# A two-layer feed-forward part behind local attention: the up projection by seven products of half blocks

## The reference

```python
# attention, B=4, H=8, S=576, D=64: pooled attention over groups of 4 positions,
# repeated 4 times, plus attention over the band |i-j| < 4
x = attn_out.transpose(0, 2, 1, 3).reshape(2304, 512)
h = x @ w_in                    # 512 -> 2048
g = np.where(h > 0.0, h, np.exp(np.minimum(h, 0.0)) - 1.0)
x = g @ w_out                   # 2048 -> 512
h = x @ w_in2                   # 512 -> 2048
r = np.maximum(h, 0.0)
out = (s * (r * r) + b) @ w_out2
```

## Time and profile before

| | us |
|---|---|
| median of 3 runs (lowest, highest) | 928.75 (927.66, 928.97) |
| the profiled execution | 932.17 |
| its span | 930.4 |
| PE busy in the span | 905.8 |
| DVE, ACT, POOL busy | 396.3, 413.1, 148.3 |

### The profile page before, as it was taken

One profiled execution on the slowest core, in us unless ns is written; L12 is line 12 of the kernel. 1 busy time (PEld: TensorE's weight loads), 2 busy tenths in 40 slices (PEclk: granted clock), 3 DMA queues, 4 the chain that ended last, 5 costly groups with the idle time before them and its releaser, 6 DMA issues.

```text
span 930.4 us, 16164 instructions
## 1 busy us (share of the span) xinstructions
PE 905.8 (97%) x5936; PEld 853.6 (92%) x5936; DVE 396.3 (43%) x774; ACT 413.1 (44%) x1104; POOL 148.3 (16%) x148
## 2 busy tenths in 40 slices
PE   5898999999999999999999999999999999999998
PEld 5777789999999999999999989899998999999896
DVE  6788844233233233232333453443443443443433
ACT  8889976544344343344466432232232332322222
POOL 5565647300000000000156400000000000000000
PEclk9889999999999999999999999999999999999999
DMA  8987534200000000000044200000000000000000
GB/s 196 206 199 195 131 100 135 62 1 1 1 0 0 0 0 0 0 1 1 23 125 125 69 1 0 35 1 1 35 0 0 34 0 0 35 1 1 34 1 35
DMA packets 42929, 41.47 MB, mean 45 GB/s; under 512 B 3616, under 2 KB 30080, under 8 KB 42880
## 3 DMA queue, kind: packets, MB, share of 16 engines
q1 hardware_dynamic: 42880, 40.83, 16.7%
HBM read 36.09 MB, written 4.72 MB: 44 GB/s over the span
## 4 chain that ended last, share of the span: by engine, by line
PE 90%; SPq 2%; issue 2%; POOL 2%; DVE 2%; ACT 1%; DMA 1%; POOLq 0%; ACTq 0%; DVEq 0%
PE ps_h L517 43%; PE ps_y L538 22%; PE ps_y L536 21%; PE ps_t L450 1%; PE ps_sd L435 1%; POOL v L371 1%; SPq L243 1%; PE ps_xd L479 1%; PE ps_s L426 1%; ACT prob L568 1%; DMA wstage<-in_w_in 1%; PE ps_x L470 1%; DVE prob L700 0%; POOL q_half L364 0%; POOL qd L366 0%
## 5 line engine op out<-in xcount | busy, mean ns | idle before, releaser
L660 ACT ACTIVATE g_hi<-tmp 128x384 fp32r<-128x384 f32 x192 | 101.0, 526 | 262.5 <-PE ps_y L538 153.1
L654 ACT ACTIVATE tmp<-ps_h 128x384 f32<-128x384 f32 x192 | 94.2, 490 | 227.2 <-PE ps_h L517 224.7
L804 DVE TENSOR_TENSOR g_lo<-tmp,g_hi 128x384 fp32r<-128x384 f32 x192 | 107.4, 559 | 205.4 <-ACT g_hi L660 205.4
L517 PE MATMUL ps_h<-xs_hi,win_late_lo 128*128 128x384 f32 x576 | 193.8, 336 | 0.0
L517 PE MATMUL ps_h<-xs_hi,win_late_hi 128*128 128x384 f32 x576 | 193.8, 336 | 0.0
L517 PE MATMUL ps_h<-xs_lo,win_late_hi 128*128 128x384 f32 x576 | 193.6, 336 | 0.0
L796 DVE SCALAR_TENSOR_TENSOR tmp<-tmp,ps_h 128x384 f32<-128x384 f32 x96 | 53.2, 554 | 162.1 <-ACT tmp L657 161.2
L517 PEld LDWEIGHTS ps_h<-xs_lo,win_late_hi 128*128 128x128 f32 x576 | 108.3, 188 | 3.3
L517 PEld LDWEIGHTS ps_h<-xs_hi,win_late_hi 128*128 128x128 f32 x576 | 108.3, 188 | 3.2
L517 PEld LDWEIGHTS ps_h<-xs_hi,win_late_lo 128*128 128x128 f32 x576 | 108.3, 188 | 0.0
L800 DVE TENSOR_TENSOR tmp<-tmp 128x384 f32<-128x384 f32 x96 | 55.2, 575 | 121.1 <-ACT tmp L654 121.1
(11 more groups left out here) (87 smaller groups left out, 1435.9 us busy)
## 6 DMA issues: line engine op xcount, KB each, us to landing
wstage<-in_w_in SPq DMA_DIRECT2D x32, 256.0 KB, 2.8
wstage<-in_w_out SPq DMA_DIRECT2D x32, 256.0 KB, 2.8
...
```

The lines of the kernel that those rows point to most:

```text
L517: mm = pe.matmul(o, w_chunk(0, a, j)[:, c * P:(c + 1) * P], xs[x][:, slot, c, :], start=(c == 0 and p == 0), stop=(c == CH - 1 and p == 2))
L654: act.activation(x, ps_h[:, j % 4, 0:TB], ACT.Relu, scale=-1.0 if layer == 0 else 1.0).then_inc(relu_ready, 1)
L660: act.activation(g[0][:, j % 2, :], x, ACT.Copy).then_inc(hi_ready, 1)
L804: dve.tensor_tensor(g[1][:, j % 2, :], x, g[0][:, j % 2, :].bitcast(F32), ALU.subtract).then_inc(g_ready, 1)
```

## The change

It leaves the attention's arithmetic as it is and rewrites the feed-forward part.

Tokens go in 3 blocks of 768 (`TB`), features in 8 groups of 256 (`FP`), which makes 48 slots (2 layers by 3 blocks by 8). In a slot the up projection is a 2x2 by 2x2 product of half blocks: tokens in halves of 384 (`TH`), the model dimension in halves of 256, features in halves of 128 (`f`). Seven products stand for eight: the four sums of x (`sum_x`, into `xsum`) once per block, the four sums of the weights (`sum_w_in`, into `wsum`) once per group and layer, and the seven sums of the products per slot (`add`, on DVE, into `hsum`; the first product is copied there by ACT, `copy_product`). Each product is 6 matmuls of 384 columns (2 chunks by 3 terms) into one of now two `ps_h` banks, where the eight half-block products before were 48 matmuls. `ps_y` has six banks. In layer 0 the down projection of 768 columns is cut into pieces of 512 and 256 columns (`y_pieces`), in layer 1 it is 36 matmuls of 512 columns a slot.

PE's order in a slot is P0 P1 U P2 U P3 U P4 U P5 U P6 and the rest of the U, where P is a product of this slot and U a unit of the down projection of the slot before (8 units a slot in layer 0, 6 in layer 1). Each product waits until DVE or ACT has taken the one two before it out of its bank (`h_added`, `h_copied`). Relu, exp, minus one and max, square, hi and lo of g work on 768 columns; the affine goes to ACT.

SBUF has room for two groups' split weights, not for a layer's. hi and lo of the seven weight operands (0.92 MB each) are made once per group in a layer's first block, stored to DRAM (`keep_w_in`, `wc_kept`) and fetched again in the two other blocks (`fetch_w_in`, two slots ahead). `w_out` is loaded and split in every slot (`lo_w_out`), on ACT and DVE. POOL does nothing after attention. The splits of early weight chunks and their loads leave the attention pipeline; in its last two steps (`left` 1 and 0) the first group's sums and splits come in, on DVE and on ACT. The weights are laid out on the host so that each group is one run per partition.

The names `hi_x`/`lo_x`, `hi_w_in`/`lo_w_in`, `hi_w_out`/`lo_w_out`, `hi_g`/`lo_g` are the two parts of each split, hi on ACT and lo on DVE, each over 768 (x, g, second part of w_in) or 1024 columns. `elu_max`, `relu_square` are DVE operations over 768 columns. The diff, cut (removed bodies and helpers left out, indentation shortened):

```diff
-    TB = 384
+    TB = 768
+    TH = TB // 2
     NB = TOK // TB
...
+    FP = w_in0.shape[1]
+    SLOTS = 2 * NB * FP
     NO = TB // P
+    KO = 2 * P
...
+    ORDER = (1, 6, 7, 5, 3, 4, 2)
+    PROD = len(ORDER)
+    X_SLOT = {k: i for i, k in enumerate(ORDER)}
+    SUMMED = (5, 6, 7, 3)
+    W_SLOT = {5: 0, 6: 1, 7: 2, 4: 3, 2: 4, 1: 5, 3: 6}
+    WS = len(SUMMED)
+    NADD = 7
...
+xsum = keep("xsum", [P, len(SUMMED), 2, TH])
+xs = [keep(f"xs_{x}", [P, PROD, 2, TH], F32R) for x in ("hi", "lo")]
+wstage = [keep(f"wstage{i}", [P, 2, 1024]) for i in range(2)]
...
+    wc = [sbb(f"wc_{x}", [P, 2, PROD, KO], F32R) for x in ("hi", "lo")]
+    wsum = sbb("wsum", [P, WS, KO])
+    wo = [sbb(f"wo_{x}", [P, 2, 2, DM], F32R) for x in ("hi", "lo")]
+    g = [sbb(f"g_{x}", [P, 2, 2, TB], F32R) for x in ("hi", "lo")]
+    hsum = sbb("hsum", [P, 2, 2, TB])
+    act_out = sbb("act_out", [P, 2, TB])
+    ps_h = second.enter_context(nc.psum_tensor("ps_h", [P, 2, 512], F32))
+    ps_y = second.enter_context(nc.psum_tensor("ps_y", [P, NO, 512], F32))
...
+wc_kept = nc.dram_tensor("wc_kept", (2, FP, 2, P, PROD * KO), F32, kind="Internal").ap()
...
-    with eng.Fori(0, B - 1) as n:
+    with eng.Fori(0, B - 2) as n:
         for u in range(CH):
...
+            body(n, u, PAIRS)
+    for n in range(B - 2, B):
+        for u in range(CH):
+            body(n, u, PAIRS - 1 - (n * CH + u))
...
+def is_split(sl):
+    return sl % (NB * FP) < FP
...
+def y_pieces(c):
+    cut = 512 if c % 2 == 0 else 256
+    return [(c * TB, 0, cut), (c * TB + cut, cut, TB)]
...
+    def keep_w_in(sl):
+        sp.wait_ge(w_split[0], split_number(sl) + 1)
+        for x in range(2):
+            sp.dma_start(wc_kept[layer_of(sl), sl % FP, x],
+                         wc[x][:, sl % 2].rearrange("p k x -> p (k x)").bitcast(F32)).then_inc(wc_stored[sl % 2], 16)
+    def fetch_w_in(sl):
+        sp.wait_ge(prod_ready, PROD * (sl - 1))
+        if is_split(sl - 2):
+            sp.wait_ge(wc_stored[sl % 2], 32 * (split_number(sl - 2) // 2 + 1))
+        for x in range(2):
+            sp.dma_start(wc[x][:, sl % 2].rearrange("p k x -> p (k x)").bitcast(F32),
+                         wc_kept[layer_of(sl), sl % FP, x]).then_inc(wc_loaded[sl % 2], 16)
...
-        if u == 0:
-            for half in range(2):
-                sp.wait_ge(w_split[half], n + 1)
-                load_w(0, n, half, 0)
         if left >= 3:
             sp.wait_ge(values_ready, i + 1)
             load_v(n + (u + 3) // CH, (u + 3) % CH)
+        if left == 4:
+            load_w_in(0)
+        if left == 3:
+            load_w_out(0)
+        if left == 2:
+            load_w_in(1)
+            load_w_out(1)
...
+    keep_w_in(0)
+    load_w_in(2)
+    for sl in range(SLOTS):
+        if sl % FP == 1 and block_of(sl) > NB:
+            store(block_of(sl) - 1)
+        if sl + 2 < SLOTS:
+            load_w_out(sl + 2)
+        if sl + 1 < SLOTS and is_split(sl + 1):
+            keep_w_in(sl + 1)
+        if sl + 3 < SLOTS and is_split(sl + 3):
+            load_w_in(sl + 3)
+        if sl + 2 < SLOTS and not is_split(sl + 2):
+            fetch_w_in(sl + 2)
+    store(2 * NB - 1)
...
-        if u in W_TURNS:
-            lo_w(0, n, W_TURNS.index(u), 0, early=True)
...
+    def product(sl, pos):
+        k = ORDER[pos]
+        made = PROD * sl + pos
+        if pos == 0:
+            if is_split(sl):
+                pe.wait_ge(w_split[0], split_number(sl) + 1)
+            else:
+                pe.wait_ge(wc_loaded[sl % 2], 32 * (fetch_number(sl) // 2 + 1))
+        if sl % FP == 0:
+            pe.wait_ge(x_split, PROD * block_of(sl) + pos + 1)
+        if made < 2:
+            pe.wait_ge(masked, PAIRS)
+        elif pos == 2:
+            pe.wait_ge(h_copied, sl + 1)
+        else:
+            was, at = divmod(made - 2, PROD)
+            pe.wait_ge(h_added, NADD * was + (None, 1, 2, 4, 5, 6, 7)[at])
+        o = ps_h[:, made % 2, 0:TH]
+        for c in range(2):
+            for q, (a, x) in enumerate(((0, 0), (0, 1), (1, 0))):
+                mm = pe.matmul(o, wc[a][:, sl % 2, W_SLOT[k], c * P:(c + 1) * P], xs[x][:, X_SLOT[k], c, :],
+                               start=(c == 0 and q == 0),
+                               stop=(c == 1 and q == 2))
+        mm.then_inc(prod_ready, 1)
...
+        layer, blk, p = layer_of(sl), block_of(sl), sl % FP
+        units = CH if layer == 0 else NO // 2
+        f = 1 - unit // units
+        if unit == 0:
+            pe.wait_ge(w_split[1], sl + 1)
+        if unit % units == 0:
+            pe.wait_ge(g_ready, 2 * sl + 2 - f)
+        u = unit % units
+        first, last = p == 0 and f == 1, p == FP - 1 and f == 0
+        if first:
+            if blk == 0:
+                pe.wait_ge(x_ready, PAIRS + 1)
+            elif layer == 0:
+                pe.wait_ge(act_evac if u < 2 else dve_evac, evac_count(blk))
+            else:
+                if u < 2:
+                    pe.wait_ge(act_evac, evac_count(blk))
+                if u > 0:
+                    pe.wait_ge(dve_evac, evac_count(blk))
...
+        if layer == 0:
+            for q, (a, x) in enumerate(((0, 0), (0, 1), (1, 0))):
+                for o, start, end in y_pieces(u):
+                    mm = pe.matmul(ps_yf[:, o:o + end - start], wo[a][:, sl % 2, f, u * P:(u + 1) * P],
+                                   g[x][:, sl % 2, f, start:end],
...
+    for sl in range(SLOTS):
+        units = 0 if sl == 0 else 2 * CH if layer_of(sl - 1) == 0 else NO
+        between = (0, 1, 1, 1, 1, 1, 0)
+        if sl == SLOTS - 1:
+            between = (0, 1, 0, 1, 0, 1, 0)
+        done = 0
+        for pos in range(PROD):
+            product(sl, pos)
+            for unit in range(done, min(done + between[pos], units)):
+                down(sl - 1, unit)
+            done = min(done + between[pos], units)
+        for unit in range(done, units):
+            down(sl - 1, unit)
+    for unit in range(NO):
+        down(SLOTS - 1, unit)
...
+    def hi_w_in(sl, part):
+        i = split_number(sl)
+        if part == 0:
+            act.wait_ge(w_sum, i + 1)
+            if sl >= 2:
+                act.wait_ge(prod_ready, PROD * (sl - 1))
+                if is_split(sl - 2):
+                    act.wait_ge(wc_stored[sl % 2], 32 * (i // 2))
+            act.activation(w_part(0, sl, 0, WS), wsum[:], ACT.Copy).then_inc(w_hi[0], 1)
+        else:
+            w = wstage[i % 2][:, 0, 0:3 * KO].rearrange("p (k x) -> p k x", x=KO)
+            act.activation(w_part(0, sl, WS, PROD), w, ACT.Copy).then_inc(w_hi[0], 1)
...
-        if u in W_TURNS:
-            hi_w(0, n, W_TURNS.index(u), 0, n + 1, True)
+        if left == 1:
+            hi_x(0, 1)
         act.wait_ge(dvalues_ready, i + 1)
         act.activation(xd[:], ps_xd[:, 0:SD], ACT.Copy).then_inc(xd_copied, 1)
         if left >= 2:
             exp_band(n2, u2, first_tiles)
-        early_split(split_x, left)
+        if left == 1:
+            hi_w_in(0, 0)
+            hi_w_in(0, 1)
     pairs(act, step)
...
+    act.wait_ge(sb_loaded, 32)
+    for k in (6, 7, 5, 3):
+        hi_x(0, k)
...
+        act.wait_ge(prod_ready, PROD * sl + 1)
+        if sl >= 2:
+            act.wait_ge(act_ready, 2 * (sl - 2) + 2)
+        act.activation(hsum[:, sl % 2, 0, 0:TH], ps_h[:, PROD * sl % 2, 0:TH], ACT.Copy).then_inc(h_copied, 1)
...
+        copy_product(sl)
+        if sl >= 1:
+            hi_g(sl - 1, 0)
+        if p == 0:
+            hi_x(blk, 4)
+        hi_w_out(sl)
+        if p == 0:
+            hi_x(blk, 2)
+        if split_next:
+            hi_w_in(sl + 1, 0)
+        if refill:
+            hi_x(blk + 1, 1)
+        if split_next:
+            hi_w_in(sl + 1, 1)
+        if refill:
+            hi_x(blk + 1, 6)
+            hi_x(blk + 1, 7)
+        middle(sl, 1)
+        if refill:
+            hi_x(blk + 1, 5)
+        hi_g(sl, 1)
+        if refill:
+            hi_x(blk + 1, 3)
+        middle(sl, 0)
+        if p == 0 and blk > 0:
+            evacuate(blk - 1)
...
+        if i == 0:
+            dve.wait_ge(scores_ready, PAIRS)
+            dve.wait_ge(dscores_ready, PAIRS)
+        else:
+            dve.wait_ge(w_sum_used, i)
+        w = wstage[i % 2][:, 0, :].rearrange("p (k x) -> p k x", x=KO)
+        b10, b00, b11, b01 = (w[:, x, :] for x in range(4))
+        dve.tensor_tensor(wsum[:, 0, :], b01, b00, ALU.subtract).then_inc(w_part_sum, 1)
+        dve.tensor_tensor(wsum[:, 2, :], b11, b01, ALU.subtract)
+        dve.wait_ge(w_part_sum, 2 * i + 1)
+        dve.tensor_tensor(wsum[:, 1, :], b11, wsum[:, 0, :], ALU.subtract).then_inc(w_part_sum, 1)
+        dve.wait_ge(w_part_sum, 2 * i + 2)
+        dve.tensor_tensor(wsum[:, 3, :], wsum[:, 1, :], b10, ALU.subtract).then_inc(w_sum, 1)
...
+        if left == 1:
+            sum_x(0, 5)
+            sum_x(0, 6)
+            sum_w_in(0)
+        if left == 0:
+            lo_w_in(0, 0)
+            lo_w_in(0, 1)
+            lo_x(0, 1)
```

(56 more changed lines are left out.)

461 lines of the change are left out of this document (215 added, 246 removed).

## The result

The changed kernel takes **899.98 us** (median of 4 runs, 899.55 to 901.27) against 928.86 in the same comparison: a ratio of 0.970 (95% interval 0.968 to 0.972), 28.9 us less. The forecast was 23.9 less, 904.9. The profiled execution has a span of 899.1 us, 31.3 less than the 930.4 before.

The account below looks back on a forecast made before the run. The prediction took PE's matmul column count to bound the feed-forward part; -50.0 + 2.6 + 2.5 + 5.0 + 18.0 - 3.0 + 1.0 = -23.9 us, so 928.75 - 23.9 = 904.9 us, range 893 to 923.

Parts of the forecast that it names:

- part 1: Up projection: seven products for eight remove 288 matmuls at 0.1736 us each, -50.0 us.
- part 2: Layer 0's down matmuls in pieces of 512 and 256 columns: cost 0, between 0 and 33.4 us.
- part 3: Steady slot of 15.6 us: PE hides the added sums, 0 per slot, 1.0 us to spare in layer 0.
- Rival (c): Slot lacks its 1.0 us to spare: one more 0.5 us handover in 46 slots, 927.9 us; chance 13%.
- part 4: Block starts and layer boundary: queued DVE work delays PE, +2.6, +2.5 and +5.0 us (2 to 9).
- part 5: From attention's end to slot 1: PE waits behind ACT's and DVE's queues, +18.0 us (12 to 24).
- part 6: Attention: early weight splits and their loads leave it, -3.0 us, between 0 and -6.
- part 7: End of the kernel: six stores for three, +1.0 us.

Follow-up runs that it names:

- h_eighth: Changed kernel with the six matmuls of the fifth of the seven products made twice; 948.65 us, 48.7 more than the changed kernel.
- s_two: Changed kernel with DVE's lo part of g made three times ahead of every slot's first sum; 945.34 us (+45.4).
- a_load: Changed kernel with only eight loads of 256 KB put back in attention, the second group's weight loads moved behind attention; 902.47 us.

## Why the prediction held

**Bound and saving (part 1): right.** `h_eighth` gives 48.7 for 288 matmuls, the sum had 50.0.

**The pieces (part 2): right, by a small margin.** The cost was taken as 0 between 0 and 33.4; a load takes 0.115 to 0.117 us against the piece's 0.116. Pieces of 192 columns would have cost, by these numbers. The upper end was too high: 0.12 was not what a load of 96 columns needs, if loads in plain fp32 are no slower than these (no run shows that).

**The slot (part 3): right.** Room of 1.0 and 1.8 us was reckoned, 1.2 and 1.8 measured by `s_two`. Rival (c) failed since nothing of the chain was missing. The plain slot is 0.1 us wider, 5 us in all, which no step had.

**Block starts (part 4): right in kind, too large.** The mis-sized term is DVE's price. Timeline of DVE at the start of block 1:

```profile
253.91 0.95 DVE L854 TENSOR_TENSOR xs_lo<-xy,xs_hi 128x768 fp32r<-128x768 f32 x1
254.78 0.55 DVE L976 TENSOR_TENSOR hsum<-hsum,ps_h 128x384 f32<-128x384 f32 x1
255.24 1.22 DVE L892 TENSOR_TENSOR wo_lo<-wstage,wo_hi 128x1024 fp32r<-128x1024 f32 x1
256.38 0.95 DVE L854 TENSOR_TENSOR xs_lo<-xy,xs_hi 128x768 fp32r<-128x768 f32 x1
```

Instructions that stand ready behind one another start 0.87 us apart for 768 columns recorded as 0.95, 0.46 for 0.55, 1.14 for 1.22. In the kernel before DVE waited ahead of most of its work, so the recorded duration was the price; in the queues of a block start each of some ten instructions is 0.08 us cheaper, and two slots' queues add it up. At the boundary it is more: the last slot of layer 0 holds over twenty of them, reckoned as 17.8 us for a slot of 15.6. The slot at the boundary, timeline of PE (P0, then P3) and of DVE (where it has caught up, then P1's sum):

```profile
503.10 0.34 PE L535 MATMUL ps_h<-xs_hi,wc_hi 128*128 128x384 f32 x1
...
503.62 0.96 DVE L984 SCALAR_TENSOR_TENSOR act_out<-act_out,hsum 128x768 f32<-128x768 f32 x1 [0.52 <-ACT act_out L719]
...
508.57 0.55 DVE L976 TENSOR_TENSOR hsum<-hsum,ps_h 128x384 f32<-128x384 f32 x1
...
509.26 0.41 PE L535 MATMUL ps_h<-xs_hi,wc_hi 128*128 128x384 f32 x1 [0.77 <-DVE hsum L976]
```

DVE had nothing left over: it waited 0.52 us for ACT at the start of the slot. P1's sum ends at 509.12, 6.0 us into the slot, where 8.4 was reckoned; P3 waits 0.77 us, where the reckoned 8.4 against 5.2 to 5.9 made 2.5 to 3.2.

**The start (part 5): right in place and size.** 31.1 us from the last normalisation to the first down unit, forecast 30.3; to the first product it is 12.3 (122.33), forecast 10.9 (130.3 - 119.36). Two errors of size work against each other: DVE's queue ran faster than priced, and the granted clock fell when PE had been idle. That they nearly cancel is luck. Windows of the changed kernel, clock in the third column from the end:

```profile
118.00:122.00 4.00, 4.00 (x49) 3.70 (x51) 2.41 (x3) 1.55 (x6) 0.00 (x0) 0.50 0.64 258
124.40:131.40 7.00, 3.19 (x17) 2.62 (x16) 6.92 (x11) 5.32 (x7) 0.00 (x0) 0.99 0.22 83
131.40:138.10 6.70, 6.04 (x18) 5.16 (x18) 5.58 (x9) 1.69 (x2) 0.00 (x0) 0.50 0.34 103
```

From 118 to 122 the granted clock was 0.50, the 1.2 GHz level, behind PE's idle time of 7.13 us, and the first product took 2.09 us (to 124.42). Between 131.4 and 138.1 it was 0.50 again, behind 7 us in which PE was busy for 3.19. P4 starts at 133.22 and its matmuls stand 0.32 us apart (0.1736 at the other level); P5 follows 2.2 us later, P6 another 2.05, where a product takes 1.04. The sum had no term for that. POOL's conflict is in the trace: the second sum of x, beside POOL's pooling of v, is recorded with 1.90 us at 111.56, twice its 0.95, as SBUF — State Buffer in the Trainium skill ("Who interferes with whom") has it.

**Attention (part 6): the direction right, the size too small in this pair of profiles.** 3.0 was taken between 0 and 6, 9.3 measured, and 4.0 to 10.1 with the marks of all profiles; an estimate from the medians, which differ by 2.4 us less than the spans, is 6.9. The step that failed is the bound: ACT's 5 us was taken as its upper end, and the loads as nearly nothing although the chain had one in it for 5.62 us. `a_load` gives the loads the largest part. The granted clock up to the last normalisation was 0.90 before (12 to 119 us) and is 0.97 now (12 to 110). That goes with the gain; which of the two brings the other was not tested.

**The end (part 7):** 1.9 for 1.0; three copies on each engine and six stores in a row. Timeline of the end:

```profile
892.13 0.39 PE L571 MATMUL ps_y<-wo_hi,g_lo 128*128 128x512 f32 x1
...
892.56 1.89 DVE L1006 COPY xsum<-ps_y 128x512 f32<-128x512 f32 x3 [7.80 <-PE ps_y L571]
...
893.18 3.08 SPq L335 DMA_DIRECT2D out<-xsum  x6
```

The six issues take 3.08 us, where three took 1.50.
